# Expert rows stored gated and without padding, the last layer reading them in expert order, its output scattered to the tokens

## The chip, the cores and the metric

The kernel runs on one core of a Trainium2 chip. The metric is the device time of one launch in microseconds. TensorE (PE in the profile), VectorE (DVE), ScalarE (ACT), GpSimd (POOL) and the queue engine SyncE (SP) run side by side and wait for each other only at semaphores.

## What is computed

```python
def reference(...):
    attn = _attn_ref(q, k, v, proj)                      # 2 x 8 heads, 768 tokens, 64 wide
    x = attn.transpose(0, 2, 1, 3).reshape(1536, 512)    # N = 1536 tokens
    # expert layer: each token goes to one of 8 experts
    logits = x @ w_gate
    expert_idx = np.argmax(logits, axis=1)
    gate_w = softmax(logits)[token, expert_idx]
    for e in range(8):
        mask = expert_idx == e
        out[mask] = gate_w[mask, None] * (np.maximum(x[mask] @ w1[e], 0.0) @ w2[e])   # 512 -> 1024 -> 512
    # last layer: 512 -> 2048 -> 512
    h = out @ w_in
    g = np.where(h > 0.0, h, np.exp(np.minimum(h, 0.0)) - 1.0)
    return g @ w_out
```

The attention compares only tokens of equal hash bucket; that stage is not touched by the change.

## The kernel before

Every product is made of three matmuls of float32r parts (high by high, low by high, high by low), a helper called `three`.

**Attention and routing.** The attention leaves its rows in `x_rows` (12 tiles of 128 tokens). DVE then finds each token's expert, its gate and its row `pos` in a padded list of ST = 19 tiles of 128 rows, in which every expert begins at a tile of its own. GpSimd scatters the 12 tiles of `x_rows` to `x_slots` in DRAM (line 470), one indirect DMA each.

**Expert phase.** For tile t, ACT loads `xg` from `x_slots` (`load_xg`), PE turns it (`turn_xg`, line 637), makes the two halves of the hidden layer (`hidden`), turns them (`turn_hidden`, line 652), and makes the output in `ps_s[:, 2]` (`expert_out`). The phase is software-pipelined: `tile(t)` on PE is `hidden(t, 0)`, `turn_hidden(t-1, 1)`, `expert_out(t-1)` in two halves, `turn_xg(t+1)`, `turn_hidden(t, 0)`, `hidden(t, 1)`. ACT and DVE move what PE made (lines 828 to 836, and 1072 and 1078); DVE copies the output to `y_sb` (line 1085) and ACT stores it to `y_slots` (line 840). Meanwhile SP loads weights in chunks of 512 KB into four staging buffers and GpSimd splits each into `w_hi` and `w_lo` (lines 480 and 484), 8 chunks for an expert, into a ring that holds two experts. `w_ready` counts the chunks. Behind the eighth expert it splits the first half of the last layer's weights, and later the second half.

**Last layer.** It goes over NBLK = 3 blocks of 4 tiles (512 tokens). GpSimd gathers each tile from `y_slots` by `pos` (line 513), ACT scales it by the gate (line 872), PE turns it (`turn_y`, line 711), and ACT and DVE move it into `yT_hi` and `yT_lo`. Then for 16 steps f: `inner(f)` makes 128 hidden columns (12 matmuls, lines 726 to 728), DVE and ACT apply the activation and split it (`elu_e`, `gT_hi`, `gT_lo`), and `outer(f)` adds into the four banks of `ps_s` (12 matmuls). `inner` runs two steps ahead of `outer`. The turns of block b+1 are set between the steps of block b (TURN_AT); those of block 0 stand in a row ahead of its first `inner`:

```python
            for q in range(BT):
                turn_y(0, q)
            inner(0, 0, 0)
            inner(0, 0, 1)
```

SP stores the output tiles (line 379).

## Time and profile before

| | |
|---|---|
| time, median of 3 runs | 862.69 us (861.37 to 862.85) |
| the profiled execution: its time, its span | 862.61 us, 860.9 us |
| busy share of the span: PE, DVE, ACT, POOL | 91%, 47%, 40%, 44% |
| share of the chain that ended last: PE, issue, POOL, DMA, DVE | 68%, 14%, 6%, 5%, 4% |
| DMA moved | 93.87 MB |

The profiled execution's own time is 1.7 us more than its span, the time between the first and the last thing that the profile shows. The busy shares are means over three stages with different limits; the chain is the work that could not have ended sooner, followed back from the end.

### The profile page before, as it was taken

The numbers are of one execution on the slowest core, as the hardware profiler recorded it, in microseconds if no ns is written. First come the engines' busy times: TensorE is split into PE (matmuls) and PEld (weight loads), VectorE is DVE, ScalarE is ACT, GpSimd is POOL, SyncE is SP. The second block draws the span as 40 slices with busy tenths as digits, with TensorE's granted clock in tenths as the row PEclk, the third lists the DMA queues.
The fourth block names the chain that finished last, engine by engine and source line by source line (L and its number), as shares of the span: only waits on it lengthen the run. The fifth ranks groups of instructions, "written<-read, shape, count | busy, mean of one in ns | idle before, by whom it ended". The sixth has DMA issues, their size and how long they took to land.

```text
span 860.9 us, 13834 instructions
## 1 busy us (share of the span) xinstructions
PE 786.8 (91%) x4070; PEld 662.5 (77%) x4071; DVE 400.8 (47%) x696; ACT 342.2 (40%) x675; POOL 380.9 (44%) x462
## 2 busy tenths in 40 slices
PE   5899999999999319999999999959999999999998
PEld 4789988888888207888887778737888888888886
DVE  5888888887888501122212212213343443434333
ACT  5777777777778102122222122122232322222222
POOL 3334434433443179599999999149300000000000
PEclk9999999999999859999999999978999999999999
DMA  5556564454352065366566556224000100000001
GB/s 159 131 166 185 121 195 107 113 139 125 82 135 86 15 229 175 109 216 192 179 215 196 192 199 193 98 65 144 13 25 13 49 0 0 0 30 20 1 1 49
DMA packets 70732, 93.87 MB, mean 109 GB/s; under 512 B 32048, under 2 KB 34096, under 8 KB 70704
## 3 DMA queue, kind: packets, MB, share of 16 engines
q1 hardware_dynamic: 62528, 77.06, 30.6%
q10 hardware_dynamic: 6256, 10.16, 3.4%
q0 software_dynamic: 1920, 6.29, 2.2%
q8 instruction: 15, 0.25, 0.1%
q14 instruction: 13, 0.11, 0.0%
HBM read 59.54 MB, written 16.25 MB: 88 GB/s over the span
## 4 chain that ended last, share of the span: by engine, by line
PE 68%; issue 14%; POOL 6%; DMA 5%; DVE 4%; ACT 1%; SPq 1%; POOLq 1%; DVEq 0%
PE ps_s L628 9%; PE ps_s L630 9%; PE ps_s L629 9%; PE ps_t L581 6%; PE ps_t L726 5%; PE ps_t L728 5%; PE ps_t L727 5%; PE ps_o L593 4%; PE ps_o L594 4%; PE ps_s L564 3%; PE ps_s L565 3%; POOL w_lo L484 2%; POOL w_hi L480 2%; DMA late_stage<-in_moe_w_dram 2%; PE ps_p L544 2%
## 5 line engine op out<-in xcount | busy, mean ns | idle before, releaser
L795 ACT ACTIVATE probs<-ps_s,stats 128x768 f32<-128x768 f32 x96 | 95.3, 993 | 26.4 <-POOL stats L434 25.9
L965 DVE TENSOR_TENSOR pt_lo<-ps_t,pt_hi 128x384 fp32r<-128x384 f32 x192 | 97.0, 547 | 9.9 <-ACT pt_hi L788 9.6
L952 DVE TENSOR_REDUCE stats<-ps_s 128x1 f32<-128x768 f32 x96 | 91.5, 953 | 18.6 <-PE ps_s L565 18.3
L484 POOL TENSOR_TENSOR w_lo<-stage,w_hi 128x1024 fp32r<-128x1024 f32 x36 | 87.6, 2434 | 0.0
L581 PE MATMUL ps_t<-ident,probs 128*128 128x128 f32 x576 | 82.5, 277 | 5.1 <-DVE pt_lo L965 5.0
L484 POOL TENSOR_TENSOR w_lo<-late_stage,w_hi 128x1024 fp32r<-128x1024 f32 x36 | 86.9, 2435 | 0.0
L788 ACT ACTIVATE pt_hi<-ps_t 128x384 fp32r<-128x384 f32 x192 | 83.5, 490 | 7.8 <-PE ps_t L581 7.4
L432 POOL TENSOR_SCALAR stats<-stats 128x1 f32<-128x1 f32 x96 | 21.1, 220 | 145.7 <-DVE stats L952 145.6
L726 PE MATMUL ps_t<-yT_hi,w_hi 128*128 (+1 forms) x192 | 77.3, 402 | 2.2 <-DVE yT_lo L1110 1.4
L581 PEld LDWEIGHTS ps_t<-ident,probs 128*128 128x128 f32 x576 | 65.8, 140 | 16.4 <-DVE pt_lo L965 13.9
L727 PE MATMUL ps_t<-yT_lo,w_hi 128*128 (+1 forms) x192 | 76.8, 400 | 0.0
L728 PE MATMUL ps_t<-yT_hi,w_lo 128*128 (+1 forms) x192 | 76.7, 400 | 0.0
L628 PE MATMUL ps_s<-w_hi,gT_hi 128*128 128x512 f32 x192 | 76.6, 399 | 0.0
L629 PE MATMUL ps_s<-w_hi,gT_lo 128*128 128x512 f32 x192 | 75.9, 395 | 0.0
L630 PE MATMUL ps_s<-w_lo,gT_hi 128*128 128x512 f32 x192 | 75.8, 395 | 0.0
L892 ACT ACTIVATE elu_e<-elu_e 128x512 f32<-128x512 f32 x48 | 30.3, 632 | 112.3 <-DVE elu_e L1127 112.3
L564 PE MATMUL ps_s<-key_hi_hi,query_lo_hi 128*128 128x384 f32 x192 | 69.8, 364 | 4.4 <-DMA query_lo_hi<-query_hi_mask 2.3
L1078 DVE TENSOR_TENSOR hidT_lo<-ps_t,hidT_hi 128x512 fp32r<-128x512 f32 x38 | 26.1, 687 | 100.6 <-ACT hidT_hi L836 100.6
L593 PE MATMUL ps_o<-pt_hi,v_split 128*128 128x384 f32 x192 | 70.4, 367 | 1.2 <-DVE pt_lo L965 1.2
L628 PE MATMUL ps_s<-w_hi,xgT_hi 128*128 x152 | 62.8, 413 | 3.1 <-DVE xgT_lo L1072 1.7
L565 PE MATMUL ps_s<-key_lo_mask,query_hi_mask 128*128 128x384 f32 x192 | 65.2, 340 | 0.0
L594 PE MATMUL ps_o<-pt_lo,v_split 128*128 128x384 f32 x192 | 64.7, 337 | 0.0
(151 smaller groups left out, 1613.2 us busy)
## 6 DMA issues: line engine op xcount, KB each, us to landing
stage<-in_moe_w_dram SPq DMA_DIRECT2D x72, 256.0 KB, 3.0
late_stage<-in_moe_w_dram SPq DMA_DIRECT2D x56, 256.0 KB, 2.9
key_hi_hi<-query_hi_mask SPq DMA_DIRECT2D x30, 192.0 KB, 3.8
x_slots<-x_rows SPq DMA_DIRECT2D x19, 256.0 KB, 3.9
xg<-x_slots ACTq DMA_DIRECT2D x19, 256.0 KB, 3.1
y_slots<-y_sb ACTq DMA_DIRECT2D x19, 256.0 KB, 2.8
raw_qk<-in_q_dram SPq DMA_DIRECT2D x16, 192.0 KB, 3.2
raw_v<-in_v_dram SPq DMA_DIRECT2D x16, 192.0 KB, 2.6
```

What stands on the lines that cost most here:

```text
L484: g.tensor_tensor(wl[:, ds(at + c * CH, CH)], stages[c % 4].rearrange("p m f -> p (m f)"), wh[:, ds(at + c * CH, CH)].bitcast(F32), ALU.su ...
L564: mm(to, qk_lo[j][:, u * P:(u + 1) * P], key_hi[j][:, cols], start=True, stop=False)
L581: last = nc.tensor.transpose(ps_t[:, half, t * P:(t + 1) * P], probs[:, (s - 2) % 4, kt * P:(kt + 1) * P], ident[:])
L593: mm(ps_o[:, 0:HW], v2[jv][:, kt].rearrange("p a d -> p (a d)"), pt_hi[gb][:, kt], start=kt == 0, stop=False)
L594: last = mm(ps_o[:, 0:HW], v2[jv][:, kt].rearrange("p a d -> p (a d)"), pt_lo[gb][:, kt], start=False, stop=kt == QT - 1)
L628: mm(to, x_hi, wh[:, w], start=start, stop=False)
L629: mm(to, x_lo, wh[:, w], start=False, stop=False)
L630: return mm(to, x_hi, wl[:, w], start=False, stop=stop)
L726: mm(ps_t[:, f % 2], wa, ya, start=k == 0, stop=False)
L727: mm(ps_t[:, f % 2], wa, yb, start=False, stop=False)
L728: last = mm(ps_t[:, f % 2], wb, ya, start=False, stop=k == KD - 1)
L965: v_.tensor_tensor(pt_lo[gb][where], ps_t[:, half, 0:HW].rearrange("p (t c) -> p t c", c=P), pt_hi[gb][where].bitcast(F32), ALU.subtract). ...
```

## The change

Each row of `x_slots` gets two more numbers: the token's gate (column DM) and its number (column DM + 1), so a row has 514 numbers. DVE copies them for each tile to `info`, multiplies the gate in where it moves the expert output, and adds the token number, so a row of `y_dense` has 513. The store of tile t goes to a row of its own (`dense_at`, a new table that ACT reads with a register load), such that the padding of one expert is overwritten by the rows of the next: `y_dense` holds the 1536 rows in expert order without gaps. Each store waits until the one before it has landed.

The last layer takes those rows as they lie, with plain loads in place of gathers: block 0 and 1 by ACT (`load_y`, from tiles 12 and 17 of the expert phase), block 2 by SP. The scaling on ACT is gone. The turns of block 0 move to the ends of tiles 13 to 16 (TURN_IN = 13), `inner(0, 0)` moves ahead of the last `turn_hidden`, and `inner(0, 1)` behind the last `expert_out`. GpSimd, not SP, writes the output: an indirect scatter for each of the 12 tiles, by `token_of`. The loops over tiles end at tile 10, the rest and the blocks of the last layer are written out.

```diff
+    XC, YC = DM + 2, DM + 1
+    FIRST_IN = [11, 15, ST]
+    TURN_IN = 13
...
-    out_d = out.rearrange("(b p u) d -> b u p d", p=P, u=QT)
-    x_slots = nc.dram_tensor("x_slots", (ST * P, DM), F32, kind="Internal").ap()
-    y_slots = nc.dram_tensor("y_slots", (ST * P, DM), F32, kind="Internal").ap()
+    x_slots = nc.dram_tensor("x_slots", (ST * P, XC), F32, kind="Internal").ap()
+    y_dense = nc.dram_tensor("y_dense", (ST * P, YC), F32, kind="Internal").ap()
     x_slot_tiles = x_slots.rearrange("(t p) d -> t p d", p=P)
-    y_slot_tiles = y_slots.rearrange("(t p) d -> t p d", p=P)
+    y_dense_tiles = y_dense.rearrange("(t p) d -> t p d", p=P)
...
-            for t in range(TT):
-
-                sp.wait_ge(acc_moved_a if t % BT < 2 else acc_moved_v, t // BT * 2 + t % 2 + 1 + 1)
-                sp.dma_start(out_d[t // QT, t % QT], out_sb[:, t % BT]).then_inc(out_stored, 16)
-            sp.wait_ge(out_stored, 16 * TT + 16)
+            sp.wait_ge(y_out, 16 * FIRST_IN[2])
+            for q in range(BT):
+                sp.wait_ge(yT_lo_moved, BT + q + 1)
+                sp.dma_start(yg[:, q], y_dense_tiles[2 * BT + q]).then_inc(yg_in[q], 16)
+            sp.wait_ge(out_stored, 16 * TT)
...
+            pool.wait_ge(slots_clear, 16 * ST)
+            g.tensor_copy(x_rows[:, :, DM + 1], iota_i[:, m_i:m_i + TT]).then_inc(tokens_set, 1)
+            pool.wait_ge(tokens_set, 1)
...
-            pool.wait_ge(y_out, 16 * ST)
-
-            def gather(t):
-                if t >= BT:
-                    pool.wait_ge(yT_made, t - BT + 1)
-                g.indirect_dma_start(out=yg[:, t % BT], out_offset=None, in_=y_slots,
-                                     in_offset=bass.IndirectOffsetOnAxis(ap=pos[:, t:t + 1], axis=0)).then_inc(yg_in[t % BT], 16)
-
-            for t in range(BT):
-                gather(t)
-            convert(E * EC, EC * CH, behind=lambda c: gather(BT + c - 1) if 1 <= c <= BT else None)
-            for t in range(2 * BT, TT):
-                gather(t)
+            pool.wait_ge(y_made, ST + 1)
+            convert(E * EC, EC * CH)
+
+            for t in range(TT):
+
+                pool.wait_ge(y_tokens, t + 1)
+                pool.wait_ge(acc_moved_a if t % BT < 2 else acc_moved_v, t // BT * 2 + t % 2 + 1 + 1)
+                g.indirect_dma_start(out=out, out_offset=bass.IndirectOffsetOnAxis(ap=token_of[:, t:t + 1], axis=0),
+                                     in_=out_sb[:, t % BT], in_offset=None).then_inc(out_stored, 16)
...
+                if isinstance(t, int) and 0 <= t - TURN_IN < BT:
+                    turn_y(0, t - TURN_IN, ps_p)
+
+            def turn_y(blk, q, bank):
 
                 n = blk * BT + q
-                pe.wait_ge(yg_scaled, n + 1)
-                if not (isinstance(blk, int) and blk == 0 and q < 2):
-                    pe.wait_ge(yT_lo_moved, n - 1)
+                pe.wait_ge(yg_in[q], blk * 16 + 16)
...
-                pe.wait_ge(g_lo, m + 1)
+                if blk == 0 and f < 2:
+                    pe.wait_ge(hidT_lo_moved, ST * 2 - 1 + f)
+                else:
+                    pe.wait_ge(g_lo, m - 1)
...
+                        if blk == 0 and q == 2:
+                            pe.wait_ge(y_moved, ST)
...
+            for t in range(UNROLLED_FROM + 1, ST):
+                tile(t, t % 2, last=t == ST - 1)
+            inner(0, 0)
+            turn_hidden(ST - 1, 1)
+            pe.wait_ge(w_ready, (E - 1) * EC + W_START)
+            slab = (expert(ST - 1) % 2) * (EC * CH)
+            for half in range(2):
+                expert_out(ST - 1, half, slab)
+            inner(0, 1)
+            for blk in range(NBLK):
                 layer(blk)
...
+                row = act.value_load(dense_at[0:1, ds(t, 1)], min_val=0, max_val=ST * P - P)
+                if not (isinstance(t, int) and t == 0):
+                    act.wait_ge(y_out, t * 16)
                 act.wait_ge(y_moved, t + 1)
-                act.dma_start(one(y_slot_tiles, t), y_sb[:]).then_inc(y_out, 16)
+                act.dma_start(y_dense[ds(row, P)], y_sb[:]).then_inc(y_out, 16)
+
+            def load_y(blk):
+
+                act.wait_ge(y_out, FIRST_IN[blk] * 16)
+                for q in range(BT):
+                    if blk:
+                        act.wait_ge(yT_lo_moved, (blk - 1) * BT + q + 1)
+                    act.dma_start(yg[:, q], y_dense_tiles[blk * BT + q]).then_inc(yg_in[q], 16)
...
                 if not last:
+                    act.wait_ge(xg_lo, t + 1)
                     load_xg(t + 1)
+                if isinstance(t, int) and t == TURN_IN - 1:
+                    load_y(0)
+                if isinstance(t, int) and t == TURN_IN + BT:
+                    load_y(1)
...
             move_hidT(ST - 1, 1)
+            steps(0, 0, 1)
             store_y(ST - 1)
-
-
-            def scale_yg(t, q, turn):
-
...
+            padding, padded = small[:, 2, 0:E], spare[:, 0]
+            step(v_.scalar_tensor_tensor(padding, filled, float(P), et[5][:, :, TT - 1], ALU.mult, ALU.subtract))
+            step(v_.tensor_tensor(te_fit, te_fit, padding.rearrange("p (o e) -> p o e", o=1).to_broadcast([P, ST, E]), ALU.mult))
+            step(v_.tensor_reduce(padded, te_fit, AX.X, ALU.add))
+            step(v_.scalar_tensor_tensor(spare[:, 1], tv[:], float(P), padded, ALU.mult, ALU.subtract))
...
+                if not (isinstance(t, int) and t < 2):
+                    dve.wait_ge(y_moved, t - 1)
+                v_.tensor_copy(info[:, odd], xg[:, DM:XC])
...
-            def move_y(t, start=False):
-                dve.wait_ge(y_made, t + 2)
+            def move_y(t, odd, start=False):
+                dve.wait_ge(xg_lo, t + 1)
                 if not start:
                     dve.wait_ge(y_out, t * 16)
-                v_.tensor_copy(y_sb[:], ps_s[:, 2]).then_inc(y_moved, 1)
+                v_.tensor_copy(y_sb[:, DM:YC], info[:, odd, 1:2])
+                dve.wait_ge(y_made, t + 2)
+                v_.tensor_scalar(y_sb[:, 0:DM], ps_s[:, 2], info[:, odd, 0:1], None, ALU.mult).then_inc(y_moved, 1)
...
+            def turn_move(blk, q, bank):
+                n = blk * BT + q
+                dve.wait_ge(yT_hi_moved, n + 1)
+                v_.tensor_copy(token_of[:, n:n + 1], yg[:, q, DM:YC]).then_inc(y_tokens, 1)
+                v_.tensor_tensor(yT_lo[blk % 2][:, :, q * P:(q + 1) * P], bank[:].rearrange("p (k c) -> p k c", c=P),
+                                 yT_hi[blk % 2][:, :, q * P:(q + 1) * P].bitcast(F32), ALU.subtract).then_inc(yT_lo_moved, 1)
...
+            steps(0, 0, 1)
+            move_y(ST - 1, (ST - 1) % 2)
+            steps(0, 1, NF)
+            for blk in range(1, NBLK):
+                steps(blk, 0, NF)
```

The first place is PE's program between the experts and the last layer. Before, the rows from the last matmul of the last `hidden` (L630 on xgT) to the first `inner` (L726) are:

```order
L630 MATMUL ps_s<-w_lo,xgT_hi 128x512
L652 MATMUL ps_t<-ident,hid 128x128 x4
L624 TENSOR_LOAD expert_of
...
L630 MATMUL ps_s<-w_lo,hidT_hi 128x512
L711 MATMUL ps_o<-ident,yg 128x128 x4
L711 MATMUL ps_p<-ident,yg 128x128 x4
L711 MATMUL ps_o<-ident,yg 128x128 x4
L711 MATMUL ps_p<-ident,yg 128x128 x4
L726 MATMUL ps_t<-yT_hi,w_hi 128x512
```

In the changed program (L636 is the same matmul as L630 before, L658 is `turn_hidden`, L720 to L722 are `inner`):

```order
L636 MATMUL ps_s<-w_lo,xgT_hi 128x512
L720 MATMUL ps_t<-yT_hi_113,w_hi 128x512
L721 MATMUL ps_t<-yT_lo_114,w_hi 128x512
...
L722 MATMUL ps_t<-yT_hi_113,w_lo 128x512
L658 MATMUL ps_t<-ident,hid 128x128 x4
L630 TENSOR_LOAD expert_of
...
L636 MATMUL ps_s<-w_lo,hidT_hi 128x512
L720 MATMUL ps_t<-yT_hi_113,w_hi 128x512
```

The four turns are gone from this place; 12 matmuls of `inner` stand ahead of the last `turn_hidden`, and the last `expert_out` is followed by `inner` at once.

The second place is ACT's program for one tile of the expert phase. Before:

```order
L824 DMA xg<-x_slots 128x512
L832 ACTIVATE hid<-ps_s 128x512
L836 ACTIVATE hidT_hi<-ps_t 128x512
L828 ACTIVATE xgT_hi<-ps_o 128x512
L836 ACTIVATE hidT_hi<-ps_t 128x512
L840 DMA y_slots<-y_sb 128x512
L832 ACTIVATE hid<-ps_s 128x512 x2
```

In the changed program, at tile 12:

```order
L832 DMA xg<-x_slots 128x514
L859 DMA yg<-y_dense 128x513 x4
L840 ACTIVATE hid<-ps_s 128x512
L844 ACTIVATE hidT_hi<-ps_t 128x512
L836 ACTIVATE xgT_hi<-ps_o 128x512
L844 ACTIVATE hidT_hi<-ps_t 128x512
L847 TENSOR_LOAD dense_at
L847 ISA x2
L851 ISA
L851 DMA y_dense<-y_sb 128x513
L840 ACTIVATE hid<-ps_s 128x512
```

A register load and its checks come ahead of every store, and tile 12 (and 17) issues four loads ahead of `hid`.

The third place is the end of GpSimd's program. Before, from the last chunk of the first half of the layer's weights on:

```order
L484 TENSOR_TENSOR w_lo<-late_stage,w_hi 128x1024 x2
L513 DMA yg<-y_slots,pos 128x512 x4
L480 TENSOR_SCALAR w_hi<-stage 128x1024 x2
L484 TENSOR_TENSOR w_lo<-stage,w_hi 128x1024
...
L513 DMA yg<-y_slots,pos 128x512 x4
```

In the changed program, the same rows and the end:

```order
L496 TENSOR_TENSOR w_lo<-late_stage,w_hi 128x1024 x2
L492 TENSOR_SCALAR w_hi<-stage 128x1024 x2
L496 TENSOR_TENSOR w_lo<-stage,w_hi 128x1024
...
L496 TENSOR_TENSOR w_lo<-late_stage,w_hi 128x1024 x2
L525 DMA out_dram<-out_sb,token_of 1536x512 x12
```

The 12 gathers are gone, and 12 scatters of output tiles stand at the end.

## Rows read from the trace of the kernel before

**Rows 1.** Windows: busy time by engine, then PE clock, DMA share, GB/s

```profile
core 0: us, PE busy (x) PEld busy (x) DVE busy (x) ACT busy (x) POOL busy (x), PEclk, DMA share, GB/s
321.00:560.00 239.00, 235.53 (x1109) 190.46 (x1110) 49.24 (x74) 51.74 (x93) 210.31 (x124) 0.99 0.55 179
567.00:591.00 24.00, 13.01 (x42) 9.41 (x43) 5.92 (x9) 6.24 (x11) 19.08 (x15) 0.64 0.41 126
591.00:855.00 264.00, 264.00 (x1149) 212.66 (x1148) 104.14 (x152) 69.92 (x114) 19.97 (x14) 1.00 0.05 18
```

**Rows 2.** Timeline of PE between experts and last layer: start, duration

```profile
558.85 0.40 PE L630 MATMUL ps_s<-w_lo,xgT_hi 128*128 x1
559.93 0.66 PE L652 MATMUL ps_t<-ident,hid 128*128 128x128 f32 x4 [0.69 <-ACT hid L832]
560.89 0.49 PE L628 MATMUL ps_s<-w_hi,hidT_hi 128*128 x1 [0.30 <-issue]
566.36 0.39 PE L630 MATMUL ps_s<-w_lo,hidT_hi 128*128 x1
581.62 0.79 PE L726 MATMUL ps_t<-yT_hi,w_hi 128*128 128x512 f32 x1 [1.41 <-DVE yT_lo L1110]
590.47 0.49 PE L726 MATMUL ps_t<-yT_hi,w_hi 128*128 x1 [0.81 <-DVE gT_lo L1131]
```

**Rows 3.** Chain that ended last, over the same stretch: start, us

```profile
567.51 2.82 DMA y_slots<-y_sb
...
574.47 3.83 DMA yg<-y_slots,pos
...
586.89 0.70 DVE elu_e L1127
...
589.64 0.70 DVE gT_lo L1131
...
604.73 0.44 PE ps_o L711 x4
```

**Rows 4.** Timeline of PE and POOL in the expert phase

```profile
465.25 0.60 PE L637 MATMUL ps_o<-ident,xg 128*128 128x128 f32 x4
...
493.56 2.44 POOL L484 TENSOR_TENSOR w_lo<-stage,w_hi 128x1024 fp32r<-128x1024 f32 x1
...
496.29 0.49 PE L628 MATMUL ps_s<-w_hi,xgT_hi 128*128 x1 [1.14 <-POOL w_lo L484]
...
510.42 4.81 POOL L484 TENSOR_TENSOR w_lo<-late_stage,w_hi 128x1024 fp32r<-128x1024 f32 x2
...
515.37 0.49 PE L628 MATMUL ps_s<-w_hi,hidT_hi 128*128 x1 [0.26 <-POOL w_lo L484]
...
537.42 4.79 POOL L484 TENSOR_TENSOR w_lo<-late_stage,w_hi 128x1024 fp32r<-128x1024 f32 x2
```

**Rows 5.** DMA issues of the weight loads: count, size, median us to landing

```profile
stage<-in_moe_w_dram SPq DMA_DIRECT2D x72, 256.0 KB, 3.0
```

**Rows 6.** Timeline of ACT in tile 14

```profile
506.43 0.40 ACTq L840 DMA_DIRECT2D y_slots<-y_sb  x1
...
509.12 0.60 ACT L832 ACTIVATE hid<-ps_s 128x512 f32<-128x512 f32 x1 [2.17 <-PE ps_s L630]
```

**Rows 7.** Timeline of the last output tiles

```profile
855.65 1.30 ACT L883 ACTIVATE out_sb<-ps_s 128x512 f32<-128x512 f32 x2 [2.84 <-PE ps_s L630]
...
856.28 2.53 SPq L379 DMA_DIRECT2D out_dram<-out_sb  x4
...
857.05 1.39 DVE L1119 COPY out_sb<-ps_s 128x512 f32<-128x512 f32 x2 [3.52 <-PE ps_s L630]
```

**Rows 8.** Timeline of gathers on POOL: the first and fourth of four

```profile
570.60 1.06 POOL L513 DMA_INDIRECT yg<-y_slots,pos  x1 [28.38 <-DMA y_slots<-y_sb]
...
574.47 0.95 POOL L513 DMA_INDIRECT yg<-y_slots,pos  x1 [0.30 <-issue]
```

**Rows 9.** Chain that ended last, from the last scatter to the first tile

```profile
312.26 2.71 DMA x_slots<-x_rows,pos
314.99 3.78 DMA xg<-x_slots
```

**Rows 10.** The queue of the 24 indirect DMAs: packets, MB, engine share

```profile
q0 software_dynamic: 1920, 6.29, 2.2%
```

More of the change, by code:

```diff
@@ L857, in tile @@
                 move_hid(t, 1)
+                if isinstance(t, int) and 0 <= t - TURN_IN < BT:
+                    turn_move(0, t - TURN_IN, ps_p)
             tile(0, 0, first=True)
-            with act.Fori(0, (ST - 3) // 2) as pair:
+            tile(1, 1)
+            tile(2, 0)
+            with act.Fori(1, UNROLLED_FROM // 2) as pair:
                 tile(pair * 2 + 1, 1)
                 tile(pair * 2 + 2, 0)
-            tile(ST - 2, 1)
-            tile(ST - 1, 0, last=True)
+            for t in range(UNROLLED_FROM + 1, ST):
+                tile(t, t % 2, last=t == ST - 1)
@@ L904, in _ @@
-            for q in range(BT):
-                scale_yg(q, q, 16)
-                if q > 0:
-                    turn_move(0, 0, q - 1)
-            turn_move(0, 0, BT - 1)
-            layer(0, first=True)
-            with act.Fori(1, NBLK - 1) as blk:
-                layer(blk)
-            layer(NBLK - 1, last=True)
+            steps(0, 1, NF)
+            for blk in range(1, NBLK):
+                steps(blk, 0, NF)
             move_outputs(NBLK - 1)
@@ L1037, in _ @@
             step(v_.tensor_scalar(small[:, 3, 0:TT], total, 1e-9, None, ALU.add))
-            step(v_.reciprocal(gate[:], small[:, 3, 0:TT]))
+            step(v_.reciprocal(x_rows[:, :, DM], small[:, 3, 0:TT]))
             dve.wait_ge(rt_count, 2)
@@ L1117, in move_outputs, with steps @@
                     dve.wait_ge(acc_made, blk * BT + q + 1)
-                    dve.wait_ge(out_stored, blk * (16 * BT) + 16)
+                    if blk:
+                        dve.wait_ge(out_stored, blk * (16 * BT))
                     v_.tensor_copy(out_sb[:, q], ps_s[:, q]).then_inc(acc_moved_v, 1)
-            def layer(blk, first=False, last=False):
-                for f in range(NF):
-                    if f == 1 and not first:
+            def steps(blk, first, end):
+                for f in range(first, end):
+                    if f == 1 and blk > 0:
                         move_outputs(blk - 1)
@@ L1139, in _ @@
             dve.sem_inc(acc_moved_v, 1)
-            dve.sem_inc(out_stored, 16)
-            for q in range(BT):
-                turn_move(0, 0, q)
-            layer(0, first=True)
-            with dve.Fori(1, NBLK - 1) as blk:
-                layer(blk)
-            layer(NBLK - 1, last=True)
+            steps(0, 0, 1)
+            move_y(ST - 1, (ST - 1) % 2)
+            steps(0, 1, NF)
+            for blk in range(1, NBLK):
+                steps(blk, 0, NF)
             move_outputs(NBLK - 1)
```

178 lines of the change are left out of this document (82 added, 96 removed).

## Prediction

> **What bounds the kernel now.** I read the windows by stage first, then PE's timeline at the seams, then the chain. From 591 to 855 us PE is never idle, at a granted clock of 1.00, so the last layer itself can't give or lose anything except by work put on PE [rows 1]. From 321 to 560 PE is busy 235.5 of 239 us [rows 1]. The one large hole is the seam between the two: in 567 to 591 PE is busy 13.0 of 24 us and its clock falls to a mean of 0.64 [rows 1]. PE's last expert matmul starts at 566.36, the first `inner` at 581.62, and the third `inner`, from where on nothing stops PE, at 590.47 [rows 2]. The chain tells what fills it: the store of the last tile, four gathers, scaling, turns and moves, and then, behind two `inner`s, the activation of step 0, from 586.89 to 590.34 [rows 3]. A second limit lies under the expert phase: GpSimd's splitting. At 496.29 and 515.37 PE waits for a chunk [rows 4]; it splits the eight chunks of the layer's first half between 515.23 and 542.21, 3.37 us each [rows 4].
>
> **The seam.** I lay out PE's new order with PE's own durations. The 24 matmuls of the last `expert_out` start from 560.89 to 566.36, and the first of them is 0.10 longer than the others (0.49 against 0.39), so matmuls of 512 columns follow each other every (5.47 - 0.10) / 23 = 0.2335 us [rows 2]. A dozen is 2.80 us, `expert_out` with 24 is 5.61 us. The last `hidden` matmul starts at 558.85, so the next may start at 559.09 [rows 2]. From there: `inner(0, 0)` 2.80, `turn_hidden` 0.44 (four transposes at full clock, as the 0.44 of a turn [rows 3]), `expert_out` 5.61, `inner(0, 1)` 2.80, hence `inner(0, 2)` at 559.09 + 11.65 = 570.74. Before, it started at 590.47 [rows 2]: 19.73 us less. Nothing should hold this sequence up. The first half of the layer's weights is split by 542.21 [rows 4], 17 us ahead. `inner(0, 0)` hides the 0.69 us in which PE waited for `hid` [rows 2]. The activation of step 0 takes 3.45 us [rows 3] and now runs beside `expert_out`'s 5.61; that of step 1 (3.45) runs beside `inner(0, 2)` and `outer(0, 0)` (5.61). The second half of the weights starts on GpSimd when PE has ended the experts, some 569; four chunks later is 583, and they are wanted by `inner(0, 8)` six steps of 5.61 on, at 604. The slow clock goes too, as PE has no pause left here.
>
> **The turns of block 0** are work moved, not removed: 4 x 0.44 = 1.76 us into tiles 13 to 16. The one at the end of tile 13 falls just ahead of 496.29, where PE waits 1.14 us for GpSimd [rows 4], and is free. The one of tile 14 lies ahead of 515.37; the printed idle there is 0.26, and as a matmul of 0.39 us lets the next start after 0.23, the real gap is 0.42 [rows 4]: practically free. Behind it GpSimd is no longer waited for, so tiles 15 and 16 pay 0.88. Bounds 0 and 1.76. The seam nets 19.73 - 0.88 = 18.85.
>
> **The tail.** Before, the first of the last four output tiles is in `out_sb` at 856.28, the last at 857.05 + 1.39 = 858.44, and the store that follows ends the span at 860.9 [rows 7]. Now GpSimd issues four scatters in a row. Four gathers start 3.87 us apart from first to last [rows 8], and GpSimd woke 0.27 us after what it waited for (567.51 + 2.82 = 570.33 to 570.60) [rows 3, 8]. So the fourth scatter starts at 856.28 + 0.27 + 3.87 = 860.42 on the old clock. From start to landing a scatter took 2.71 [rows 9], a gather 3.83 [rows 3]. A scatter is a scatter: 863.13, a loss of 2.23; with the gather's figure 3.35. The earlier eight scatters lie beside PE's layer and cost nothing.
>
> **Wider rows.** 2,056 in place of 2,048 bytes is 0.4% of bytes, and the two landings that lie open are the last scatter, 2.71, and the first `xg`, 3.78 [rows 9]: between 0 and a few tenths; I take 0.3. A tile takes PE 48 matmuls and three sets of four transposes, 48 x 0.2335 + 3 x 0.44 = 12.5 us, and the later `xg` loads and the stores have most of that as cover.
>
> The Trainium skill, DMA: Bandwidth & Descriptors, section How a descriptor splits into AXI transactions, speaks against such rows: a descriptor that does not start on a 256-byte boundary fetches from the boundary below, so a 2,056-byte row may need ten transactions where 2,048 aligned bytes need eight. By that a quarter of the transfer time would come on top; as an estimate from the page alone that is under 1 us on these two landings, and no run here shows it yet.
>
> **ACT and DVE.** ACT's tile gets a register load ahead of the store. In tile 14 the store is issued at 506.43 and done by 506.83 with the move of `hidT_hi` beside it until 506.95, and ACT's next work comes at 509.12 [rows 6]. That leaves 2.2 us free, and `hid` is wanted only after the next `hidden` half, 2.80 - 0.60 = 2.2 us later, 4.4 in all. The load has no duration in this trace, but PE does two such loads per tile without a visible pause; I take 0. The four loads at tile 12 cost four issues of 0.40, 1.6 us, inside 2.2. If that cover were gone the excess would come once or twice. The three small DVE steps of a tile come in an engine that is busy 49 of 239 us [rows 1]: 0. The wait for the store before, now also on ACT, is for something issued a whole tile of 12.5 us earlier that lands in 2.82 [rows 3]: 0. The five new routing steps run while GpSimd scatters: 0. The scaling on ACT was off PE's path except in the seam: nothing more.
>
> **Weight loads beside the y loads.** Four tiles are 1.05 MB. The phase moves 179 GB/s at a share of 0.55 [rows 1], so 146 GB/s are left and the burst lasts 7 us. Weight loads land in 3.0 us [rows 5] and are issued two chunks, 6.7 us, ahead of use with two issues of 0.4 us each: 2.9 us in hand. Doubled to 6 they would come at the moment they are used. I take 0, with 3 as the upper bound; it would count in full only for block 0's burst near 480, while GpSimd still sets PE's pace.
>
> **Sum.** -18.85 + 2.23 + 0.3 = -16.3. Against the profiled execution's 862.61 this is 846.3 us; the median of the runs is 862.69, so nothing is to be added.
>
> **Rivals.** Weights late: the y burst stalls GpSimd by up to 3 us and the landings are the gather's (1.1 more): 849 to 853. For it speaks that GpSimd is without pause there; against it the 2.9 us in hand. 0.14.
>
> Rows of 2,056 bytes cost GpSimd twice the pieces. The 24 indirect DMAs show 1,920 packets, 80 each, for 128 rows [rows 10]: 64 of two rows and 16 others would fit. If a row no longer fits the scheme and the 12 scatters of `x_rows`, which lie open, took 0.95 us more each (the duration of one [rows 8]), 11.4 us come back: 857.7, or 853 to 860. 0.07.
>
> More is gained: all four turns vanish in waits and the tail is as short as before: 846.3 - 0.9 - 2.2 = 843.2. 0.09.
>
> Slower: ACT's register load. If load and checks held ACT longer than the 4.4 us above in each tile, PE would wait for `hid` in all 18 tiles. It decides from 4.4 + 16.3 / 18 = 5.3 us on; at 6 us it costs 29 and the kernel takes 875. Against it speaks that PE's two loads per tile leave no trace. 0.05.
>
> No change at all, by a mixture near that point: 0.03.
>
> The Trainium skill, Runtime: NRT & Kernel Launch, section Instruction fetch mechanics, says that a taken branch breaks the sequential prefetch, by which writing out the last tiles and blocks would gain more. The trace does not agree: the edges of the layer's loop lie between 591 and 855, where PE's idle time is 0.00 [rows 1].
>
> **How the numbers follow.** The forecast, 844 to 849, has 0.62; its range takes in 0 to 1.76 for the turns and 2.23 to 3.35 for the tail, and a few tenths for the rows. With the late weights and the upper part of "more", 843.3 to 852 holds about 0.8. This kernel's measurement can tell some 0.2%, 1.7 us, from no change. Faster has 0.62 + 0.14 + 0.07 + 0.09 = 0.92, the same 0.03, slower 0.05.
>
> **What would show it.** After: PE without a gap of over 0.5 us between the last expert tiles and the layer, `inner`'s third step some 11.7 us behind the last `hidden`, clock 1.00 there; transposes of `yg` in tiles 13 to 16, with the wait before tile 14 shortened by 0.44; GpSimd's w_lo without a pause between 355 and 540; four scatters about 1.3 us apart at the end and a span end some 4.7 us behind the last move into `out_sb` in place of 2.5. A pause of GpSimd near 480 for staging, a first `xg` load issued over 1 us later than 314.99, or PE waits for `hid` in every tile would make the prediction wrong.

## The result, and the profile after

The changed kernel takes 946.28 us (median of 5 runs, 943.33 to 960.15), the kernel before 862.69 (861.14 to 862.85). The ratio is 1.097, with a 95% interval of 1.095 to 1.098: 9.7% slower, where the prediction had 846.3 us and gave slower a chance of 0.05. The profiled execution is the slowest of the five, of 960.15 us with a span of 958.4: a kernel has a second, slower state in some of its executions, which adds some per cent, and the pattern below is read again from ordinary executions in the experiments. That slower was given 0.05 was for another mechanism, ACT's register load.

The busy row of the page, and two of its groups of instructions (busy us, mean ns | idle before, releaser):

```profile
PE 800.2 (83%) x4070; PEld 674.8 (70%) x4071; DVE 514.7 (54%) x751; ACT 334.6 (35%) x664; POOL 379.6 (40%) x464
...
L634 PE MATMUL ps_s<-w_hi,xgT_hi 128*128 x152 | 70.6, 464 | 95.6 <-DVE xgT_lo L1097 95.6
L1096 DVE COPY info<-xg 128x2 f32<-128x2 f32 x19 | 112.0, 5895 | 34.7 <-ACT xgT_hi L836 34.7
```

PE, whose share was 91%, stands at 83%. What is new in its idle time, 95.6 us, lies ahead of one group, the first matmuls of `hidden`, and it is DVE that is late. The second group tells why: a copy of two numbers per partition, `info[:, odd]` from `xg`, takes 5.9 us in the mean and 112 us in all.

Windows of the expert phase, the seam and the last layer, as in [rows 1]:

```profile
core 0: us, PE busy (x) PEld busy (x) DVE busy (x) ACT busy (x) POOL busy (x), PEclk, DMA share, GB/s
324.00:663.00 339.00, 243.92 (x1078) 196.36 (x1079) 162.33 (x115) 51.83 (x94) 209.40 (x125) 0.85 0.43 132
672.00:690.00 18.00, 18.00 (x81) 14.51 (x81) 6.84 (x11) 4.29 (x7) 8.16 (x6) 1.00 0.16 55
700.00:945.00 245.00, 245.00 (x1066) 197.75 (x1065) 98.08 (x150) 60.15 (x98) 16.79 (x13) 1.00 0.04 14
```

The whole loss lies in the expert phase: PE is busy 243.9 of 339 us there and its granted clock is 0.85, where [rows 1] had 235.5 of 239 and 0.99. Seam and last layer are without a pause at a clock of 1.00. Now DVE's timeline over one tile, then GpSimd's in the same stretch:

```profile
358.34 0.17 DVE L1096 COPY info<-xg 128x2 f32<-128x2 f32 x1 [0.31 <-ACT xgT_hi L836]
...
370.84 0.43 DVE L1096 COPY info<-xg 128x2 f32<-128x2 f32 x1 [0.31 <-ACT xgT_hi L836]
...
377.98 0.14 DVE L1110 COPY y_sb<-info 128x1 f32<-128x1 f32 x1
382.27 0.75 DVE L1112 TENSOR_SCALAR y_sb<-ps_s,info 128x512 f32<-128x512 f32 x1 [4.16 <-PE ps_s L636]
383.34 13.73 DVE L1096 COPY info<-xg 128x2 f32<-128x2 f32 x1 [0.32 <-ACT xgT_hi L836]
396.99 0.68 DVE L1097 TENSOR_TENSOR xgT_lo<-ps_o,xgT_hi 128x512 fp32r<-128x512 f32 x1
```

```profile
370.20 2.07 POOL L492 TENSOR_SCALAR w_hi<-stage 128x1024 fp32r<-128x1024 f32 x2 [24.68 <-PE ps_s L636]
372.23 2.41 POOL L496 TENSOR_TENSOR w_lo<-stage,w_hi 128x1024 fp32r<-128x1024 f32 x1
...
391.40 1.04 POOL L492 TENSOR_SCALAR w_hi<-late_stage 128x1024 fp32r<-128x1024 f32 x1
392.41 4.63 POOL L496 TENSOR_TENSOR w_lo<-late_stage,w_hi 128x1024 fp32r<-128x1024 f32 x2
409.07 2.06 POOL L492 TENSOR_SCALAR w_hi<-stage 128x1024 fp32r<-128x1024 f32 x2 [12.02 <-PE ps_s L636]
```

With GpSimd idle (at 358) the copy takes 0.17 us. At 383.34 it starts inside a run of GpSimd that goes without a pause from 370.20 to 392.41 + 4.63 = 397.04, and it ends at 383.34 + 13.73 = 397.07. The one-column copy of L1110 at 377.98, inside the same run, takes 0.14. A long copy of 13.7 us comes once in each of the six runs of eight chunks from 370 to 593. Behind it stands `xgT_lo`, since DVE works in order, and PE waits for that:

```profile
397.86 0.79 PE L634 MATMUL ps_s<-w_hi,xgT_hi 128*128 x1 [11.95 <-DVE xgT_lo L1097]
```

The loss feeds on itself. While PE stands, nobody frees the ring of weights, so GpSimd later pauses too (12.02 us ahead of 409.07) and then again runs eight chunks in one piece, beside a PE that has fallen behind.

The seam is as forecast. PE's timeline there, where the last `hidden` matmul, the two early `inner`s, the last `turn_hidden` and the third `inner` start:

```profile
672.53 0.40 PE L636 MATMUL ps_s<-w_lo,xgT_hi 128*128 x1
672.76 0.39 PE L720 MATMUL ps_t<-yT_hi,w_hi 128*128 128x512 f32 x1
...
675.56 0.60 PE L658 MATMUL ps_t<-ident,hid 128*128 128x128 f32 x4
...
681.59 0.39 PE L720 MATMUL ps_t<-yT_hi,w_hi 128*128 128x512 f32 x1
...
684.38 0.40 PE L720 MATMUL ps_t<-yT_hi,w_hi 128*128 128x512 f32 x1
```

From the last `hidden` to the third `inner` it is 11.85 us, where [rows 2] has 590.47 - 558.85 = 31.62. And the tail, ACT's two last moves and GpSimd's four last scatters:

```profile
949.31 1.30 ACT L870 ACTIVATE out_sb<-ps_s 128x512 f32<-128x512 f32 x2 [2.86 <-PE ps_s L636]
...
950.68 0.96 POOL L525 DMA_INDIRECT out_dram<-out_sb,token_of  x1 [79.36 <-ACT out_sb L870]
...
954.48 0.96 POOL L525 DMA_INDIRECT out_dram<-out_sb,token_of  x1 [0.30 <-issue]
```

The first of the two moves ends half-way, at 949.96, and the first scatter starts 0.72 us behind it, the fourth 3.80 us after the first, and 3.92 us behind the fourth's start the span ends, at 958.4.

### The profile page after: what moved, and what is told of

Its sections match the earlier page's. It is cut to its first block, busy times and chain, and to the rows that moved or that the text cites. A ratio compares the mean times of both kernels' runs of the same rounds, so it can differ in the third digit from the quotient of the medians.

```text
span 958.4 us, 13841 instructions
## 1 busy us (share of the span) xinstructions
PE 800.2 (83%) x4070; PEld 674.8 (70%) x4071; DVE 514.7 (54%) x751; ACT 334.6 (35%) x664; POOL 379.6 (40%) x464
## 3 DMA queue, kind: packets, MB, share of 16 engines
q0 software_dynamic: 1920, 6.31, 1.7%
## 4 chain that ended last, share of the span: by engine, by line
PE 74%; DVE 10%; issue 10%; DMA 2%; POOL 1%; ACT 1%; DVEq 0%; SPq 0%; POOLq 0%
PE ps_s L634 12%; PE ps_s L635 12%; PE ps_s L636 12%; DVE info L1096 6%; PE ps_t L587 6%; PE ps_t L720 5%; PE ps_t L722 5%; PE ps_t L721 5%; PE ps_o L599 3%; PE ps_o L600 3%; PE ps_s L570 2%; PE ps_s L571 2%; PE ps_p L550 2%; PE ps_t L658 1%; PE ps_p L535 1%
## 5 line engine op out<-in xcount | busy, mean ns | idle before, releaser
L634 PE MATMUL ps_s<-w_hi,xgT_hi 128*128 x152 | 70.6, 464 | 95.6 <-DVE xgT_lo L1097 95.6
L1096 DVE COPY info<-xg 128x2 f32<-128x2 f32 x19 | 112.0, 5895 | 34.7 <-ACT xgT_hi L836 34.7
L634 PEld LDWEIGHTS ps_s<-w_hi,xgT_hi 128*128 128x128 f32 x152 | 32.8, 216 | 105.8 <-issue 99.0
L525 POOL DMA_INDIRECT out_dram<-out_sb,token_of x12 | 11.6, 968 | 234.8 <-ACT out_sb L870 232.1
L967 DVE TENSOR_REDUCE stats<-ps_s 128x1 f32<-128x768 f32 x96 | 91.6, 954 | 19.8 <-PE ps_s L571 19.5
L492 POOL TENSOR_SCALAR w_hi<-stage 128x1024 fp32r<-128x1024 f32 x36 | 37.5, 1053 | 148.5 <-PE ps_s L636 148.4
L840 ACT ACTIVATE hid<-ps_s 128x512 f32<-128x512 f32 x38 | 22.7, 598 | 198.2 <-PE ps_s L636 194.0
L496 POOL TENSOR_TENSOR w_lo<-stage,w_hi 128x1024 fp32r<-128x1024 f32 x36 | 85.5, 2374 | 0.0
L636 PE MATMUL ps_s<-w_lo,gT_hi 128*128 128x512 f32 x192 | 76.0, 396 | 0.0
L722 PE MATMUL ps_t<-yT_hi,w_lo 128*128 128x512 f32 x192 | 76.0, 396 | 0.0
L720 PE MATMUL ps_t<-yT_hi,w_hi 128*128 128x512 f32 x192 | 76.0, 396 | 0.0
L721 PE MATMUL ps_t<-yT_lo,w_hi 128*128 128x512 f32 x192 | 75.9, 395 | 0.0
```

What stands on the lines that cost most here:

```text
L496: g.tensor_tensor(wl[:, ds(at + c * CH, CH)], stages[c % 4].rearrange("p m f -> p (m f)"), wh[:, ds(at + c * CH, CH)].bitcast(F32), ALU.su ...
L634: mm(to, x_hi, wh[:, w], start=start, stop=False)
L636: return mm(to, x_hi, wl[:, w], start=False, stop=stop)
L720: mm(ps_t[:, f % 2], wa, ya, start=k == 0, stop=False)
L721: mm(ps_t[:, f % 2], wa, yb, start=False, stop=False)
L722: last = mm(ps_t[:, f % 2], wb, ya, start=False, stop=k == KD - 1)
```

## Experiments

My theory after the trace: DVE's copy and GpSimd's splitting want the same way into SBUF, and DVE gets none while GpSimd goes on. The Trainium skill, SBUF — State Buffer, section Who interferes with whom, says that a DVE copy in a two-port mode, or a DVE operation with two inputs in SBUF beside a GpSimd instruction that reads SBUF, wants a pair of ports that GpSimd uses too, and that the one that issues second is blocked until the other's instruction is over. The trace agrees on who blocks whom and differs on how long: 13.7 us are eight of GpSimd's instructions, the longest of them 2.4 us. The Trainium skill, VectorE: DVE Perf Modes, section Mode 2×_2P, lets a float32 copy from SBUF to SBUF use both ports if its outermost dimension of more than one element is even, or odd and equal in source and destination. That one column has no such dimension and so nothing to split is my reading of it; the 0.14 us of L1110 agree.

**Two copies of one column (e1_two_copies).** Only the copy's form changes; the same two numbers arrive.

```diff
-                v_.tensor_copy(info[:, odd], xg[:, DM:XC])
+                for col in range(2):
+                    v_.tensor_copy(info[:, odd, col:col + 1], xg[:, DM + col:DM + col + 1])
```

> The changed kernel, with the one DVE copy of two columns (gate and token number) to info replaced by two copies of one column each. Port theory: the copy of two float32 columns from SBUF to SBUF runs in a mode that needs the SBUF ports DVE shares with GpSimd, and gets them only when GpSimd has a pause; a one-column copy (the 0.14 us copy to y_sb) does not. Then each copy takes 0.14 to 0.17 us, PE waits for xgT_lo in one place only, and the time is 848 us (846.3 forecast, and about 1.5 more for the tail, whose last landing took 3.9 in place of 2.71). Rival, the waits: move_xg now waits for y_moved or for xg to land, whatever the copy is: the time stays at 946. Rival, wide rows: weight loads or x loads are slower with 2,056-byte rows: 940 or more.

848.85 us (847.51 to 851.12), ratio to before 0.985 (0.983 to 0.986). The copies, then the expert phase, in its trace (ns minimum, median, maximum; windows as above):

```profile
L1097 DVE COPY info<-xg x38: 142/150/158, 321.2 to 547.1; 128x1 f32<-128x1 f32 x38
```

```profile
321.00:560.00 239.00, 235.22 (x1118) 191.23 (x1119) 56.86 (x138) 53.23 (x97) 211.50 (x125) 0.99 0.62 188
560.00:585.00 25.00, 25.00 (x111) 20.16 (x111) 9.13 (x15) 5.98 (x10) 14.46 (x9) 1.00 0.23 82
```

No copy is held any more and PE is as busy as in [rows 1]. One line of DVE's code was worth 946.3 - 848.9 = 97 us. Everything else that the change does is in this kernel too, and comes to -14 us.

**The copy alone, in the kernel before (e2_before_copy2, e3_before_copy1x2).** Nothing of the change but two numbers copied per tile to a place that nobody reads, once as one copy, once as two.

```diff
                 dve.wait_ge(xg_hi, t + 1)
+                v_.tensor_copy(info[:, odd], ident[:, 0:2])
```

> The kernel before, with one thing added: in each tile, ahead of xgT_lo, DVE copies two float32 columns of the constant ident to a spare tile that nobody reads. Port theory: eight or so of the 19 copies last 11 to 14 us, to the end of GpSimd's run of eight chunks, and the time is 950 to 970 (862.7 plus the 95.6 us that PE waited for xgT_lo in the changed kernel, less the waits on GpSimd that this replaces). Rivals (new semaphore waits, wide rows, store order): none of them is in this kernel, so 863 to 864.

> The kernel before, with two copies of one float32 column each in the same place as in the kernel before it. Port theory: 0.14 us each, hidden, 862.7 to 863.5. If any SBUF to SBUF copy on DVE beside GpSimd waits, whatever its width: 950 or more, as with two columns.

932.59 us (930.44 to 944.68), ratio 1.080 (1.078 to 1.081), and 861.10 (860.00 to 862.64), ratio 0.999 (0.998 to 1.000). From the trace of the first (of its execution of 944.68 us), the copies and PE's waits for `xgT_lo` (us in all, times, the longest):

```profile
L1073 DVE COPY info<-ident x19: 169/445/27884, 320.9 to 627.5; 128x2 f32<-128x2 f32 x19
```

```profile
PE ps_s L629 <- DVE xgT_lo L1074: 82.0, 4, 26.1
```

So the copy does it without the wider rows, the gate or the new stores. It cost less than expected: only three copies were held for long, but those for 27.8 to 27.9 us, since here GpSimd went through 16 chunks in one piece. Each began some 25.7 us into such a run of 53.5 us and ended with it. The length of a hold follows what is left of GpSimd's run, not an instruction.

**Another instruction with the same form (e4_tensor_tensor).** The two numbers made by a `tensor_tensor` whose two inputs both lie in SBUF.

```diff
-                v_.tensor_copy(info[:, odd], xg[:, DM:XC])
+                v_.tensor_tensor(info[:, odd], xg[:, DM:XC], xg[:, DM:XC], ALU.max)
```

> The changed kernel, with the two-column copy made a tensor_tensor maximum of the same two columns with themselves, which has no mode of two results per cycle but reads two SBUF inputs. If only the double-rate mode of the copy needs the shared ports, 848 us. If a second SBUF input needs the shared read port too, as the Trainium skill states in SBUF: State Buffer, it waits for GpSimd as the copy did: 940 to 950.

946.15 us (943.77 to 957.80), ratio 1.102 (1.096 to 1.107): the same loss.

```profile
L1096 DVE TENSOR_TENSOR info<-xg x19: 160/439/13774, 321.1 to 641.9; 128x2 f32<-128x2 f32 x19
```

```profile
PE ps_s L634 <- DVE xgT_lo L1097: 84.1, 8, 12.1
```

It isn't only the operation copy that waits. DVE's big subtractions, which read one side from PSUM, take 0.68 us all along. A `tensor_tensor` of one column was not run, so of this form it is shown that it is held, not that one column would let it go.

This trace, of an execution of 943.77 us with a span of 942.1, serves for the sum against the version with two copies (span 847.1). The busy rows of the two pages, this version first:

```profile
PE 795.5 (84%) x4070; PEld 671.1 (71%) x4071; DVE 503.3 (53%) x751; ACT 334.5 (36%) x664; POOL 380.6 (40%) x464
```

```profile
PE 780.1 (92%) x4070; PEld 660.0 (78%) x4071; DVE 406.9 (48%) x770; ACT 334.0 (39%) x664; POOL 381.6 (45%) x464
```

PE waits 84.1 us for `xgT_lo`, against 1.8 there, and no longer the 2.2 us that it waits there for chunks and the 0.2 for `hid`: 79.9 more. The same matmuls (x4070) take 795.5 - 780.1 = 15.4 us longer, at a granted clock of 0.86 instead of 0.99 between 324 and 560. Together that is 95.3 us, and the spans differ by 95.0.

**The copy kept, but behind the work that PE waits for (e7_copy_behind).**

```diff
-                    act.wait_ge(xg_lo, t + 1)
+                    act.wait_ge(info_in, t + 1)
                     load_xg(t + 1)
...
-                v_.tensor_copy(info[:, odd], xg[:, DM:XC])
                 v_.tensor_tensor(xgT_lo[:, odd]..., ALU.subtract).then_inc(xg_lo, 1)
+                v_.tensor_copy(info[:, odd], xg[:, DM:XC]).then_inc(info_in, 1)
```

> The changed kernel with its two-column copy, only set behind the subtraction that makes xgT_lo, not ahead of it. Port theory: the copy still waits for GpSimd's pause, and what is queued behind it on DVE is now hidT_lo of the first half, which PE wants 3.2 us later (one hidden half and one turn): nine waits shorter by 3.2, so 946 - 29 = 917. If it was the dependence of xgT_lo on the copy alone that cost, and DVE itself is free to go on: 849.

921.99 us (920.28 to 931.57), ratio 1.073 (1.068 to 1.077). DVE's timeline and PE's wait:

```profile
366.09 0.69 DVE L1097 TENSOR_TENSOR xgT_lo<-ps_o,xgT_hi 128x512 fp32r<-128x512 f32 x1 [0.32 <-ACT xgT_hi L837]
366.70 13.25 DVE L1099 COPY info<-xg 128x2 f32<-128x2 f32 x1
379.87 0.68 DVE L1104 TENSOR_TENSOR hidT_lo<-ps_t,hidT_hi 128x512 fp32r<-128x512 f32 x1
```

```profile
PE ps_s L635 <- POOL w_lo L497: 60.5, 7, 8.9
```

It is not DVE's order alone that is tried here: ACT's next load, which overwrites `xg`, now waits for the copy, and its move of `hid` stands behind that load:

```profile
380.60 0.60 ACT L841 ACTIVATE hid<-ps_s 128x512 f32<-128x512 f32 x1 [11.30 <-DVE info L1099]
```

A hold of 13.2 us is longer than the 12.5 us that a tile takes PE, so I expect no place in an in-order engine to bear it whole; no other place was run.

**What lets DVE in (e9_split_by_pairs, e11_bubbles).** In the changed kernel's trace a few copies that start in a busy GpSimd take 0.4 us: they end with the first of two hi steps (370.84 + 0.43 with 370.20 + 1.04). Does a boundary of two hi steps let DVE in? GpSimd's order by pairs of chunks gives one every 6.7 us.

```diff
-                convert_hi(0, done, at)
-                for c in range(EC):
-                    if c + 1 < EC:
-                        convert_hi(c + 1, done, at)
+                for c in range(0, EC, 2):
+                    convert_hi(c, done, at)
+                    convert_hi(c + 1, done, at)
                     convert_lo(c, done, at)
+                    convert_lo(c + 1, done, at)
```

> The changed kernel with its two-column copy kept; only GpSimd's split is issued for two chunks at a time (hi, hi, lo, lo), so that one hi step follows another about every 6.7 us. Theory A: DVE's two-column copy gets in at such a place (the copies of 0.43 us that started in a busy run of GpSimd ended there), so none waits longer than 6.7 us where it waited 13.7, PE waits up to 3 us a tile, and the time is 870 to 900. Theory B: only a pause of GpSimd lets it in; then the copies still take up to 13.7 us and the time stays at 940 to 950.

942.27 us (941.60 to 946.80), ratio 1.095 (1.092 to 1.098). Theory A has fallen. DVE's copy, and GpSimd's boundary of two hi steps that it passed by at about 367.1:

```profile
365.63 13.73 DVE L1096 COPY info<-xg 128x2 f32<-128x2 f32 x1 [0.32 <-ACT xgT_hi L836]
```

```profile
366.01 2.10 POOL L492 TENSOR_SCALAR w_hi<-stage 128x1024 fp32r<-128x1024 f32 x2
```

The next experiment gives GpSimd real pauses, short ones: within a run it waits for its own last subtraction before it goes on.

```diff
                     if c + 1 < EC:
+                        if c:
+                            wait_apart(w_ready, W_START + done + c)
                         convert_hi(c + 1, done, at)
```

> The changed kernel with its two-column copy kept; GpSimd, within a run of eight chunks, waits for its own subtraction of the chunk before ahead of each further hi step, so that it stands still for some hundredths of a microsecond at every chunk. Theory A: any moment in which GpSimd has nothing to do lets DVE in; then no copy takes longer than one chunk's 3.4 us, PE waits a fraction of it, and the time is 850 to 880. Theory B: so short a moment isn't enough, or the place is given by the run's end in another way: the copies still take 13.7 us and the time stays at 940 to 955.

862.44 us (860.39 to 865.38), ratio 1.001 (1.000 to 1.002), with the two-column copy in place. DVE and GpSimd, and the copies over the whole run:

```profile
405.01 1.61 DVE L1098 COPY info<-xg 128x2 f32<-128x2 f32 x1 [0.32 <-ACT xgT_hi L838]
```

```profile
404.21 2.39 POOL L496 TENSOR_TENSOR w_lo<-stage,w_hi 128x1024 fp32r<-128x1024 f32 x1
406.89 1.04 POOL L492 TENSOR_SCALAR w_hi<-late_stage 128x1024 fp32r<-128x1024 f32 x1 [0.29 <-POOL w_lo L496]
```

```profile
L1098 DVE COPY info<-xg x19: 168/807/2247, 320.9 to 559.4; 128x2 f32<-128x2 f32 x19
```

The copy comes through when GpSimd's instruction ends at 406.60, in a gap of 0.29 us, and none of the 19 takes longer than 2.25 us. PE waits for chunks of weights 10.8 us and for `xgT_lo` 3.0, in the version with two copies 2.2 and 1.8: 9.8 us more. Its busy time is 783.2 us instead of 780.1. Together that is 12.9 us, and the two spans differ by 12.4 (859.5 and 847.1). Most of the price is now GpSimd's pauses: 8.6 us of later chunks, against 1.2 of DVE's holds.

**The copy on ACT (e12_copy_by_act).**

```diff
                 a(xgT_hi[:, odd]..., ps_o[:], ACT.Copy).then_inc(xg_hi, 1)
+                if not (isinstance(t, int) and t < 2):
+                    act.wait_ge(y_moved, t - 1)
+                a(info[:, odd], xg[:, DM:XC], ACT.Copy).then_inc(info_in, 1)
```

> The changed kernel with the two-column copy moved from DVE to ACT, behind its move of xgT_hi. Theory: only DVE shares its way to SBUF with GpSimd, so ACT's copy takes 0.2 to 0.3 us in every tile and the time is 848 to 851, that of the version with two one-column copies (848.85). Rival: a copy of two columns is held on any engine; then it takes up to 13.7 us on ACT as well and the time is over 900.

848.27 us (847.60 to 849.99), ratio 0.984 (0.982 to 0.986).

```profile
L840 ACT ACTIVATE info<-xg x19: 191/195/205, 320.4 to 545.9; 128x2 f32<-128x2 f32 x19
```

Two columns, beside the same splitting, in 0.2 us each time: ACT is not held where DVE is.

**The other terms (e5_seam_undone, e6_plain_store).** Both start from the version with two copies. The first puts the early `inner(0, 0)` back behind the last `expert_out`, ahead of `inner(0, 1)`, which stood there already:

```diff
-            inner(0, 0)
             turn_hidden(ST - 1, 1)
...
                 expert_out(ST - 1, half, slab)
+            inner(0, 0)
             inner(0, 1)
```

> The kernel with two one-column copies, and inner(0,0) and inner(0,1) put back behind the last expert_out. The turns stay in tiles 13 to 16. If the removed gathers and turns were the whole of the seam, this costs only the wait for hid (0.69) and the part of step 0's activation (3.45) that inner(0,1) (2.80) doesn't cover, 1.4 us in all: 850.2. If the order of the two inners is what holds the seam together (clock falls again), 855 or more.

851.26 us (850.19 to 853.28), ratio 0.987 (0.986 to 0.989): 2.4 us more. PE waits where the early `inner(0, 0)` had hidden it, 0.69 for `hid` and 0.82 for `gT_lo`:

```profile
562.18 0.66 PE L658 MATMUL ps_t<-ident,hid 128*128 128x128 f32 x4 [0.69 <-ACT hid L840]
...
575.40 0.47 PE L720 MATMUL ps_t<-yT_hi,w_hi 128*128 128x512 f32 x1 [0.82 <-DVE gT_lo L1160]
```

The order of `inner` is thus worth 2.4 of the 19.8 us that the seam gives. The rest falls to the plain loads and the early turns together, by subtraction; the two were not measured apart.

The second lets SP store the tiles as they lie. It leaves out that the rows go to their tokens' places: they are written in expert order.

```diff
-                g.indirect_dma_start(out=out, out_offset=bass.IndirectOffsetOnAxis(ap=token_of[:, t:t + 1], axis=0),
-                                     in_=out_sb[:, t % BT], in_offset=None).then_inc(out_stored, 16)
+                sp.dma_start(out_d[t // QT, t % QT], out_sb[:, t % BT]).then_inc(out_stored, 16)
```

> The kernel with two one-column copies, with the output stored by SP to consecutive rows as before in place of the 12 scatters by token (the rows then stand in expert order, not in token order). The trace says that the tail behind the last move into out_sb is 6.3 us with scatters and was 2.46 with SP's stores: 848.85 - 3.8 = 845.0. If the stores are not what ends the tail, 848 to 849.

843.82 us (843.55 to 845.81), ratio 0.978 (0.977 to 0.980): 5.0 us less than with the scatters. In its trace the stretch from the last move into `out_sb` to the end is 2.4 us (841.67 to 844.1) where it was 6.3. So 3.9 us are the tail. The other 1.1 are between medians of executions that spread over 2 to 4 us, and I can't put them down to the scatters.

**A shorter tail (e8_last_two_steps, e10_steps_and_copies_behind).** The last two `outer`s of the last block run tile by tile, so that the four output tiles come 1.4 us apart and the scatters find them ready one by one.

```diff
+            def last_two(blk):
+                for q in range(BT):
+                    for f in (NF - 2, NF - 1):
...
+                        last = three(ps_s[:, q], gT_hi[:, f % 2, cols], gT_lo[:, f % 2, cols], w, False, f == NF - 1)
+                    last.then_inc(acc_made, 1)
```

> The kernel with two one-column copies, and the last two steps of the last block done output tile by output tile, so that the first tile is ready 4.2 us ahead of the last instead of 2.1. The four scatters, 1.27 us apart, then keep up with PE, and only the last one's issue and landing (0.7 + 3.9) stand behind the last move: about 2 us less, 847. If the landing of a scatter waits for the ones before it in the queue, nothing is gained: 848.8.

847.11 us (846.50 to 847.31), ratio 0.982 (0.980 to 0.984), 1.7 less than with two copies alone. The two last scatters of its trace:

```profile
840.23 0.96 POOL L525 DMA_INDIRECT out_dram<-out_sb,token_of  x1 [0.54 <-issue]
841.63 0.96 POOL L525 DMA_INDIRECT out_dram<-out_sb,token_of  x1 [0.45 <-issue]
```

The last starts 841.63 - 840.86 = 0.8 us after the last tile is in `out_sb`, so the scatters no longer queue. What is left of the tail, 845.6 - 840.86 = 4.7 us, is that start, the landing and the end of the program. With the two one-column copies set behind the subtraction as well:

> The changed kernel with two one-column copies, these set behind the subtraction that makes xgT_lo, and the last block's last two steps run tile by tile. Against the version without the move of the copies (847.11): the copies of 0.3 us stood ahead of the subtraction that PE waits for in the first tile only, so 846.8, that is no difference beyond 0.5 us, by either theory.

848.21 us (846.60 to 849.42), ratio 0.984 (0.983 to 0.986): 1.1 us more, where no difference beyond 0.5 was expected. The runs of this kernel spread over 2.8 us, and in its trace the first `hidden` starts at 323.43, in that of the version before it at 321.61: 1.8 us later, though the copies no longer stand ahead of it. So nothing is gained, and no loss is shown. The version of 847.11 us beats both the kernel before and the changed one.

## Why the prediction was wrong

**The step that failed** is "The three small DVE steps of a tile come in an engine that is busy 49 of 239 us [rows 1]: 0." The share of busy time answers whether DVE has time, not whether it may start. Two of the three steps do cost nothing; the third, two columns from SBUF to SBUF, takes up to 13.7 us in a busy run of GpSimd, and PE waits 84 to 96 us for what stands behind it. The row that spoke for it was there: GpSimd is busy 210 of the same 239 us [rows 1]. My rule for small steps should have asked of each what it reads and writes, and who holds that way. The page of the Trainium skill on SBUF named above states the conflict; by it alone (one instruction of GpSimd, 1.0 to 2.4 us) a tile would have lost up to 2.4 us, of which in `e11_bubbles`, where the holds were that short, PE felt 3.0 us in all. That a hold lasts to the end of a run was not to be had from the trace of before, in which no such copy stands; as a rival with a price between 0 and a run of GpSimd it was.

**The terms that can be held against the version with two copies**, whose profiled execution takes 848.85 us with a span of 847.1, that is 13.8 less span than before; I had 16.3.

The seam: 31.62 - 11.85 = 19.8 us, forecast 19.73. Right to 0.1, sequence and clock too, and each `inner` found its weights split.

The start: the first `hidden` begins at 322.31, in the trace of the kernel before its first L628 at 321.65. That is 0.7, where I had 0.3. The two open landings in the chain of the version with two copies, as in [rows 9]:

```profile
312.01 3.41 DMA x_slots<-x_rows,pos
315.44 3.87 DMA xg<-x_slots
```

They are 0.70 and 0.09 longer than before; the last scatter starts 0.25 earlier, so the routing steps cost nothing. This is one trace of each: in the other versions with one-column copies or the copy on ACT the first `hidden` begins between 321.53 and 323.74, so the term is no larger than what executions differ by.

The phase: mis-sized. The last `hidden` starts at 561.23, before at 558.85 [rows 2]: another 1.7, where I had 0.88 for the turns. The four turns are 1.76 us, so in effect all of them are paid for. The wait at the end of tile 13 did get shorter, 0.63 us instead of the 1.14 of [rows 4], but the one at 489.87 is 0.97 where the kernel before had 0.22 at 488.41: PE's waits for chunks are 2.2 us in all, before 1.9. What a turn hid in came back at another chunk. GpSimd had waited 0.46 us for staging at 480.55, when the y loads ran (they landed in 5.5 us, the weights in 3.0 to 3.3), which is the late-weights rival at a sixth of its upper price; that it is what lengthened the wait at 489.87 is likely, not shown.

The tail: mis-sized. From the last move into `out_sb` to the end it is 847.1 - 840.81 = 6.3 us; [rows 7] have 2.46, so it costs 3.8, where I had 2.23 and 3.35 as the upper end. The distance of the scatters was right (3.80, forecast 3.87). GpSimd's start after its wait takes 0.7, where I took 0.27 from a gather [rows 8]. The landing was right too, 2.7 us as I had it from [rows 9]. The 3.9 that my expectations for the experiments call a landing is the stretch from the last scatter's start to the end of the span. From the changed kernel's trace, the landings of the 12 scatters and SyncE's last wait behind them; then that last wait in the kernel before:

```profile
DMA to landing us min/median/max: 2.7/2.7/2.8
```

```profile
SPq L83 <- PEq L83: 1.0, 1, 1.0
```

```profile
SPq L81 <- PEq L81: 0.2, 1, 0.2
```

In that trace the last scatter starts at 954.48, so it lands at 957.2, and the span ends 1.2 us behind it, where SyncE, which had waited for the landing, waits 1.0 us more for the other engines; in the kernel before that is 0.2, and its last store, issued at 858.5, lands after 2.0, some 0.4 us ahead of the end. This end of the program is the term that I left out: I set my landing against the old span's end, as if nothing came behind it. From the first tile in `out_sb` to the end it is 0.7 + 3.8 + 2.7 + 1.3 = 8.5 us in the version with two copies, where I had 0.27 + 3.87 + 2.71 = 6.85. It is GpSimd that holds up the end: in that version's trace its closing instruction (DRAIN, L83) ends at 846.92, 1.0 us behind the landing, and the other engines' last steps start at 847.09. With SyncE's stores in place of the scatters (`e6_plain_store`) SyncE's last wait is 0.2 us again.

So -19.8 + 0.7 + 1.7 + 3.8 = -13.6, against -13.8 measured. Without the copy the forecast would have been off by 2.5 us, at the top of its own range of 844 to 849, with the turns at their upper bound and the tail beyond its own.

**Steps that were right.** ACT's register load left PE one wait for `hid` in the phase of the version with two copies, of 0.17 us in the first tile, where the kernel before had 0.25. Rows of 514 numbers did not change GpSimd's pieces: the indirect queue still has 1,920 packets, as in [rows 10]. PE never stood for the wait for the store before. With wider rows an `xg` load lands in 4.0 us instead of 3.1, a row store in 3.9 instead of 2.8 (medians of the version with two copies), under cover but for the first. In the changed kernel, with the same rows but 132 GB/s in the phase instead of 188, they are 3.4 and 3.1, so a part of it is what runs beside them. My count of ten pieces by the Trainium skill, DMA: Bandwidth & Descriptors, section How a descriptor splits into AXI transactions, was one too many: counted from a table that starts on a 256-byte boundary, each row of 2,056 bytes begins at a multiple of 8 bytes and reaches over nine, so its rule gives an eighth more and not a quarter. No run here has the rows without the rest of the change.

## What to carry to other kernels

Before you call an added small instruction free, ask three things: is its engine idle, is what it reads and writes free for it, and what stands behind it in order. On DVE a float32 copy within SBUF of two columns, or an operation of two columns with two inputs in SBUF, beside a GpSimd that works without pause, failed the second here; one column at a time, an input from PSUM, or ACT as the engine, passed. Wider forms were not tried. When a tiny instruction has a mean of 5.9 us against a minimum of 0.17, put the timeline of the other engines beside it and look which of them stops just as it ends.

## What of the hardware was not expected

DVE can be held to the end of GpSimd's run, not only of one instruction: for up to 13.7 us where a run has eight chunks (27 us), for 27.9 where it has sixteen (53.5 us). Of the 15 copies of the changed kernel's trace that took over 0.2 us, each ended either with the GpSimd instruction in which it had started (7 of them, 0.39 to 2.29 us) or, when not let in there, with the end of the run (8, of 11.33 to 13.73 us); none ended at a boundary between. With gaps of 0.3 us at every chunk none of the copies outlasted the instruction in which it started. What decides at the first boundary stays open: the copies of the version with pairs that started some 0.6 us into a run got in at its first boundary, those 13.1 us into it did not, while in the kernel before with the same copy those that started 13.2 to 13.4 us into a run did, in three runs of 16 chunks and in one of eight.
